# Attention, a token MLP and a top-1 mixture of experts: the experts' h taken to its transposed form through DRAM and VectorE, with the second product two blocks behind the first

## The chip, the cores and the metric

The kernel runs on one core of a Trainium2 chip. The metric is device time in microseconds (us) from start to end of one execution; lower is better. One core has five engines with queues of their own: TensorE (PE; its weight loads are listed as PEld), VectorE (DVE), ScalarE (ACT), GpSimd (POOL) and SyncE (SP), which here only issues DMAs. DMAs are issued from SP, ACT and POOL and move between DRAM and the on-chip memory. Matrix products land in PSUM, eight banks of 128 x 512 floats called `ps`.

## The reference

Three stages in a row on 4608 tokens of width 512.

```python
attn_out = _attn_ref(q, k, v, phi)                    # stage A
x = attn_out.transpose(0, 2, 1, 3).reshape(4608, 512)
h = x @ w_in                                          # stage B: 512 -> 2048 -> 512
x = (h / (1 + exp(-1.702 * h))) @ w_out
logits = x @ w_gate                                   # stage C: 8 experts, one for each token
e_idx = argmax(logits, axis=1)
gate_w = softmax(logits)[arange(N), e_idx]
eom = sigmoid(x @ w_output_gate)
for e in range(8):
    mask = e_idx == e
    h = maximum(x[mask] @ w1[e], 0)                   # 512 -> 1024
    out[mask] = gate_w[mask] * eom[mask, e] * (h @ w2[e])    # 1024 -> 512
```

With the inputs of this case the experts get 576, 0, 1152, 576, 1696, 576, 0 and 32 tokens; in blocks of 128 that is 5, 0, 9, 5, 14, 5, 0 and 1, 39 blocks in all.

## The kernel before

Every float32 operand of a product is split into a high and a low part (fp32r), and each product is made as high x high + high x low + low x high: three matmuls where one would do.

Stage B runs over nine tiles of 512 tokens. Beside it GpSimd splits the weights of one expert in each tile (`split_chunk`), and SP stores the parts to a DRAM scratch, `wsplit` (`store_chunk`). The tokens' results are scattered to DRAM as records of 524 floats (x, the router's numbers, the token's index), sorted by expert.

Stage C, the expert stage, runs over the 39 blocks. The busiest expert comes first (14 blocks), then the others by number: blocks 0-13, 14-18, 19-27, 28-32, 33-37 and 38. For a block i:

- GpSimd loads the records (`load_block`: four DMAs for `crec`, one for `cmeta`), VectorE transposes them in 32 x 32 blocks (`dve_x_t`), ACT and VectorE write the high and the low part `cx` (`act_x_hi`, `dve_x_lo`).
- TensorE makes h in two halves of 512 columns, 12 matmuls each (`block_h`), tokens on the partitions, in banks 0 and 1. ACT applies the relu to the first half, VectorE to the second, into `ch`.
- TensorE transposes `ch`: eight 128 x 128 transposes into banks 3 and 4 (`h_transpose`). From there ACT copies the high part and VectorE subtracts the low part, into `chT` (`act_h_hi`, `dve_h_lo`).
- TensorE makes y with 24 matmuls (`block_y`), ACT scales it by the gate (`act_y`), GpSimd scatters it to the output (`scatter_out`).

TensorE's order within block i is written out by hand: h(i), y(i-1), transposes of h(i). Every other engine has its own order, in `act_block`, `dve_block` and `pool_block`. Blocks 0 to 2 stand ahead of the loop, mixed with the end of stage B: the last tile's logits, the routing on VectorE (`route1`, `route2`), the counts, and then on VectorE some forty small instructions that make the tables of blocks, experts and rows (semaphore `b_tbl`). Records from block 3 on can only be loaded when those tables are there. Eight paddings of 128 records are stored too (`pad`), half by SP, half by ACT.

`W` has two slots of one expert's split weights each. SP loads an expert as four DMAs of 2 MB, one after the other, each waited for (`load_expert`); from the third expert on it first waits until y of the last block of the expert two before is done (`c_y`).

The functions that the diff touches follow as they were.

Of the kernel before, what the change touches and what calls it, by code (L numbers as in the profile page):

```python
# [31 lines left out]
P = 128  # L32
# [9 lines left out]
DM = H * D  # L42
# [15 lines left out]
CH = 512  # L58
EW = K1 * F2
# [31 lines left out]
def build(nc, q, k, v, phi, w_in, w_out, w_gate, w_ogate, w1, w2, cst, out):  # L91
    xT_dram = nc.dram_tensor("xT_scratch", (DM, N), F32, kind="Internal").ap()
    rec_dram = nc.dram_tensor("record_scratch", (NREC, REC), F32, kind="Internal").ap()
    wsplit = nc.dram_tensor("expert_scratch", (NE, P, 4 * EW), F32, kind="Internal").ap()
# [11 lines left out]
    with ExitStack() as ctx:  # L106
# [9 lines left out]
        sb("to_512", [P, 96])  # L116
# [14 lines left out]
        sb("to_512_again", [P, 72])  # L131
# [57 lines left out]
        with ExitStack() as a:  # L189


            sbt(a, "over_xraw", [P, K1 * T])
            ch = sbt(a, "ch", [P, F2])
            chT = sbt(a, "chT", [P, 2, C2, P], F32R)
            cy = sbt(a, "cy", [P, 2, DM])


            crec = sbt(a, "crec", [P, 4, 4, P])
            cxT = sbt(a, "cxT", [P, DM])
            cx = sbt(a, "cx", [P, 2, K1, P], F32R)  # L200
            cmeta = sbt(a, "cmeta", [P, 4, META])
            cex = sbt(a, "cex", [P, 4, NE])
            csum = sbt(a, "csum", [P, 4, 4])
# [68 lines left out]
        b_end = sem("record_ends")  # L272
        b_tbl = sem("tables")
# [7 lines left out]
        c_rec = [sem(f"records_loaded{r}") for r in range(4)]  # L281
# [4 lines left out]
        c_hact = sem("relu_by_act")  # L286
        c_hdve = sem("relu_by_dve")
# [16 lines left out]
        def ring(i, r):  # L304

            return i // 4 + 1
# [6 lines left out]
        LAST_BANK = (3, 4, 5, 6)  # L313
        EARLY = 3

# [22 lines left out]
        def blocks(eng, body, drain=None):  # L338


            n = (FULL - 3) // 4
            with eng.Fori(0, n) as m:
                for j in range(4):
                    body(4 * m + 3 + j, (3 + j) % 4)
            for i in range(3 + 4 * n, FULL):
                body(i, i % 4)
            used = eng.value_load(tbl[0:1, 5, 1:2], min_val=FULL, max_val=NBLK)
            for i in range(FULL, NBLK + 1):
                if i < NBLK:
                    with eng.If(used > i):  # L350
                        body(i, i % 4)
                if drain:
                    with eng.If(used == i):
                        drain(i, i % 4)
# [20 lines left out]
        def _(sp):  # L375
# [75 lines left out]
            def store_chunk(e, i):  # L451
                wait(sp, e_lo, 16 * e + i + 1)
                col = i * CH if i < 8 else 2 * EW + (i - 8) * CH
                for src, o in ((whi[:, i % 2, :].bitcast(F32), col), (raw[:, i % 2, :], col + EW)):
                    sp.dma_start(wsplit[bass.ds(e, 1), :, o:o + CH].rearrange("e p f -> p (e f)"), src
# [28 lines left out]
            def load_expert(e, j, chunks=range(4)):  # L484

                for n in chunks:
                    c_wn, c_n = (c_w1, 2 * j + n % 2 + 1) if n < 2 else (c_w2, 2 * j + n % 2 + 1)
                    col = n * EW
                    sp.dma_start(W[:, (j % 2) * SLOT + col:(j % 2) * SLOT + col + EW].bitcast(F32),
                                 wsplit[bass.ds(e, 1), :, col:col + EW].rearrange("e p n -> p (e n)")).then_inc(c_wn, 16)  # L490
# [1020 lines left out]
```

## Time and profile before

| | us |
|---|---|
| median of 3 runs | 1479.16 (1473.66 to 1483.98) |
| the profiled execution, its own time | 1479.53 |
| its span, first to last instruction | 1477.9 |
| TensorE busy in the span | 1407.9 (95%) |
| VectorE / ACT / GpSimd busy | 578.0 / 420.2 / 520.3 |
| stage C, from h of block 0 (993.2) to the end | 484.7 |

Starts are in us from the span's start. "L691" is line 691 of the kernel before: L691 is h, L720 is y, L731 the transposes of h, L612 and L646 are the two products of stage B. Matmuls are pipelined, so that the busy time of one (0.39 us) is longer than the distance of two starts; what a group of matmuls costs is read here from start to start. "Landing" is the time from a DMA's issue to its arrival.

### The profile page before, as it was taken

The numbers are of one execution on the slowest core, as the hardware profiler recorded it, in microseconds if no ns is written. First come the engines' busy times: TensorE is split into PE (matmuls) and PEld (weight loads), VectorE is DVE, ScalarE is ACT, GpSimd is POOL, SyncE is SP. The second block draws the span as 40 slices with busy tenths as digits, with TensorE's granted clock in tenths as the row PEclk, the third lists the DMA queues.
The fourth block names the chain that finished last, engine by engine and source line by source line (L and its number), as shares of the span: only waits on it lengthen the run. The fifth ranks groups of instructions, "written<-read, shape, count | busy, mean of one in ns | idle before, by whom it ended". The sixth has DMA issues, their size and how long they took to land.

```text
span 1477.9 us, 26796 instructions
## 1 busy us (share of the span) xinstructions
PE 1407.9 (95%) x8362; PEld 1145.9 (78%) x8363; DVE 578.0 (39%) x1254; ACT 420.2 (28%) x792; POOL 520.3 (35%) x617
## 2 busy tenths in 40 slices
PE   5777799999999999999999999998999999999997
PEld 4555578888888888888888888886888888888885
DVE  4777723334253342433334334236233233222331
ACT  3444422223222232222222322222222222222221
POOL 1121384435444344342533434013233333333332
PEclk9899999999999999999999999999999999999999
DMA  9999745555554545444453443326511265416371
GB/s 251 277 293 288 227 152 188 178 178 194 172 205 162 171 150 190 144 170 144 169 192 137 168 154 97 114 99 238 187 44 43 81 234 184 133 43 213 112 263 30
DMA packets 102359, 246.39 MB, mean 167 GB/s; under 512 B 16003, under 2 KB 16276, under 8 KB 99236
## 3 DMA queue, kind: packets, MB, share of 16 engines
q1 hardware_dynamic: 80404, 195.79, 40.3%
q0 software_dynamic: 13280, 32.09, 6.9%
q10 hardware_dynamic: 8624, 17.85, 3.5%
q8 instruction: 30, 0.49, 0.1%
q14 instruction: 21, 0.17, 0.0%
HBM read 146.00 MB, written 100.45 MB: 167 GB/s over the span
## 4 chain that ended last, share of the span: by engine, by line
PE 86%; DMA 7%; DVE 3%; SPq 2%; issue 1%; ACT 0%; POOL 0%; POOLq 0%; DVEq 0%
PE ps L612 27%; PE ps L646 26%; PE ps L691 14%; PE ps L720 14%; DMA qraw<-in_q 4%; DMA ph<-in_phi 2%; PE ps L731 2%; SPq L392 1%; PE ps L572 1%; PE ps L660 1%; PE ps L670 1%; DMA cmeta<-record_scratch 0%; PE ps L546 0%; DVE xs L1081 0%; PE ps L560 0%
## 5 line engine op out<-in xcount | busy, mean ns | idle before, releaser
L612 PE MATMUL ps<-xs,W 128*128 (+1 forms) x1728 | 422.7, 393 | 3.4 <-DVE xs L1081 3.4
L646 PE MATMUL ps<-W,gs 128*128 128x512 f32 x1728 | 415.1, 389 | 0.1
L612 PEld LDWEIGHTS ps<-xs,W 128*128 128x128 f32 x1728 | 321.6, 188 | 71.6 <-DVE xs L1081 4.0
L646 PEld LDWEIGHTS ps<-W,gs 128*128 128x128 f32 x1728 | 324.3, 188 | 67.8 <-DVE gs L1136 0.5
L1134 DVE TENSOR_TENSOR gate<-ps,gate 128x512 f32<-128x512 f32 x144 | 99.6, 691 | 401.4 <-ACT gate L887 400.9
L691 PE MATMUL ps<-W,cx 128*128 (+1 forms) x936 | 225.8, 397 | 4.7 <-DVE cx L1224 4.7
L720 PE MATMUL ps<-W,chT 128*128 (+1 forms) x936 | 218.9, 389 | 1.9 <-issue 1.9
L887 ACT ACTIVATE gate<-ps 128x512 f32<-128x512 f32 x144 | 86.1, 598 | 425.0 <-PE ps L612 412.8
L691 PEld LDWEIGHTS ps<-W,cx 128*128 128x128 f32 x936 | 174.8, 190 | 40.5 <-issue 5.2
L720 PEld LDWEIGHTS ps<-W,chT 128*128 128x128 f32 x936 | 175.6, 188 | 38.5 <-issue 2.1
L1412 POOL CAST whi<-raw 128x512 fp32r<-128x512 f32 x128 | 84.8, 663 | 305.0 <-DMA raw<-in_moe_w 304.9
L1414 POOL TENSOR_TENSOR raw<-raw,whi 128x512 f32<-128x512 f32 x128 | 172.3, 1346 | 21.5 <-POOL whi L1412 19.1
L1136 DVE TENSOR_TENSOR gs<-gate,gs 128x512 fp32r<-128x512 f32 x144 | 116.3, 808 | 100.2 <-ACT gs L891 99.5
L1426 POOL DMA_DIRECT2D crec<-record_scratch x164 | 92.4, 563 | 151.3 <-DMA out<-cy,cmeta 128.5
L891 ACT CAST gs<-gate 128x512 fp32r<-128x512 f32 x144 | 89.4, 621 | 112.8 <-DVE gate L1134 110.6
L1243 DVE TENSOR_TENSOR chT<-ps,chT 128x512 fp32r<-128x512 f32 x78 | 50.2, 686 | 180.4 <-ACT chT L934 180.3
L1467 POOL DMA_INDIRECT out<-cy,cmeta x39 | 40.6, 1041 | 166.5 <-ACT cy L941 157.3
L1420 POOL DMA_INDIRECT record_scratch<-rec,posi x36 | 36.5, 1013 | 152.4 <-DVE posi L1189 144.0
L941 ACT ACTIVATE cy<-ps,csum 128x512 f32<-128x512 f32 x39 | 26.8, 688 | 188.3 <-PE ps L720 186.8
L1238 DVE TENSOR_SCALAR ch<-ps 128x512 f32<-128x512 f32 x39 | 27.0, 691 | 105.8 <-PE ps L691 105.8
L1397 POOL CAST W<-raw 128x512 fp32r<-128x512 f32 x16 | 10.3, 644 | 132.0 <-DMA raw<-in_moe_w_in 132.0
L913 ACT CAST cx<-cxT 128x512 fp32r<-128x512 f32 x40 | 24.8, 621 | 80.3 <-PE ps L691 76.9
(159 smaller groups left out, 972.2 us busy)
## 6 DMA issues: line engine op xcount, KB each, us to landing
W<-expert_scratch SPq DMA_DIRECT2D x24, 2048.0 KB, 8.0
raw<-in_moe_w SPq DMA_DIRECT2D x128, 256.0 KB, 2.8
expert_scratch<-whi SPq DMA_DIRECT2D x128, 256.0 KB, 2.5
expert_scratch<-raw SPq DMA_DIRECT2D x128, 256.0 KB, 2.7
crec<-record_scratch POOLq DMA_DIRECT2D x164, 64.0 KB
kvm<-in_k SPq DMA_DIRECT2D x32, 288.0 KB, 5.6
kvm<-in_v SPq DMA_DIRECT2D x32, 288.0 KB, 9.8
qraw<-in_q SPq DMA_DIRECT2D x16, 576.0 KB, 14.0
```

The lines of the kernel that those rows point to most:

```text
L612: mm = pe.matmul(ps[:, f % 2, :], W[:, col:col + P], xs[:, bass.ds(x0 + (x_lo * K1 + c) * T, T)], start=(c == 0 and w_lo + x_lo == 0), sto ...
L646: mm = pe.matmul(ps[:, 2 + s, :], gs[:, f % 2, g_lo, s * P:(s + 1) * P], W[:, col:col + DM], start=(f == 0 and g_lo + w_lo == 0), stop=(f ...
L691: mm = pe.matmul(ps[:, j, :], cx[:, x_lo, c, :], W[:, bass.ds(col, 512)], start=(c == 0 and x_lo + w_lo == 0), stop=(c == K1 - 1 and x_lo ...
L720: mm = pe.matmul(ps[:, 5 + r % 2, :], chT[:, h_lo, c, :], W[:, bass.ds(col, DM)], start=(c == 0 and h_lo + w_lo == 0), stop=(c == C2 - 1 a ...
L887: act.activation(gate[:, f % 2, :], ps[:, f % 2, :], ACT.Sigmoid, scale=QTOK).then_inc(b_sig, 1)
L891: act.copy(gs[:, f % 2, 0, :], gate[:, f % 2, :]).then_inc(b_ghi, 1)
L1134: dve.tensor_tensor(gate[:, f % 2, :], ps[:, f % 2, :], gate[:, f % 2, :], ALU.mult).then_inc(b_g, 1)
L1136: dve.tensor_tensor(gs[:, f % 2, 1, :], gate[:, f % 2, :], gs[:, f % 2, 0, :].bitcast(F32), ALU.subtract).then_inc(b_glo, 1)
L1243: dve.tensor_tensor(chT[:, 1, 4 * j:4 * j + 4, :].rearrange("p c n -> p (c n)"), ps[:, 3 + j, :], chT[:, 0, 4 * j:4 * j + 4, :].rearrange( ...
L1412: pool.tensor_copy(whi[:, u, :], raw[:, u, :]).then_inc(e_hi, 1)
L1414: pool.tensor_tensor(raw[:, u, :], raw[:, u, :], whi[:, u, :].bitcast(F32), ALU.subtract).then_inc(e_lo, 1)
L1426: pool.dma_start(crec[b * M:(b + 1) * M, r], rows[:, b * P:(b + 1) * P].rearrange("(h n) d -> n h d", n=M)).then_inc(c_rec[r], 16)
```

## The change

- h goes through DRAM. The relu writes `ch` in another order of columns, `act_h_store` stores it (512 KB, 1 KB runs) to one of three places in `h_dram`, ACT waits for that, and `act_h_load` loads it back into `cq` with four tokens' quarters to a partition. VectorE transposes it in 32 x 32 blocks (`dve_h_t`, two of 512 columns) into `cqT`, from which ACT and VectorE write the parts `chT`. TensorE's eight transposes are gone.
- The second product is two blocks behind: TensorE's block is h(i), y(i-2). `chT`, `cx` and h's banks are double (banks 0, 1 and 3, 4). Before the loop the order is h0, h1, h2, y0, y1, y2, h3, h4.
- The rings of `cmeta`, `cex` and `csum` have six places, that of `crec` three; loops over blocks are unrolled by six. Record loads no longer wait for the last scatter.
- Loads of records 3 and 4 wait for a part of the tables only (`b_rows`), and stand ahead of `scatter_out(0)`. SP stores six of the eight paddings, ACT two.
- `wsplit` is laid out in pieces of 128 x 512, so that stores are contiguous and an expert's load has runs of 2 KB. SP may load w1 of a later expert when h, not y, of the old one is done.

```diff
@@ build
-    wsplit = nc.dram_tensor("expert_scratch", (NE, P, 4 * EW), F32, kind="Internal").ap()
+    wsplit = nc.dram_tensor("expert_scratch", (NE, 4, EW // CH, P, CH), F32, kind="Internal").ap()
+    h_dram = nc.dram_tensor("h_scratch", (3, 4, P, F2 // 4), F32, kind="Internal").ap()
@@ sync
-            for e in range(0, NE, 2):
+            for e in range(NE - 2):
                 pad(sp, e)
...
                         done = sp.value_load(tbl[0:1, 4, j:j + 1], min_val=1, max_val=NBLK)
+                        sp.wait_ge(c_h, done * 2)
+                    load_expert(e, j, range(2))
+                    if j >= 2:
                         sp.wait_ge(c_y, done)
-                    load_expert(e, j)
+                    load_expert(e, j, range(2, 4))
@@ tensor
             def pe_block(i, r):
-                block_h(i)
-                block_y(i - 1, (r - 1) % 4)
-                h_transpose(i)
+                block_h(i, r % 2)
+                block_y(i - 2, (r - 2) % RING)
@@ scalar
+            def act_h_store(i, n):
+                for j in range(2):
+                    wait(act, c_relu[j], i + 1)
+                act.dma_start(h_dram[n].rearrange("b p f -> p b f"), ch[:].rearrange("p (b f) -> p b f", b=4)).then_inc(c_hst, 16)
+
+            def act_h_load(i, n, u):
+                wait(act, c_hst, 16 * (i + 1))
                 wait(act, c_htr, 2 * i)
-                act.activation(ch[:, 0:512], ps[:, 0, :], ACT.Relu).then_inc(c_hact, 1)
-
-            def act_h_hi(i):
+                act.dma_start(cq[:], h_dram[n].rearrange("b (n h) f -> (b n) (h f)", h=4)).then_inc(c_hld[u], 16)
...
             def act_block(i, r):
-                act_relu(i)
+                act_relu(i, r % 2)
                 if not isinstance(i, int) or i + 1 < NBLK:
-                    act_x_hi(i + 1)
-                    act_exp(i + 1, (r + 1) % 4)
-                act_y(i - 1, (r - 1) % 4)
-                act_h_hi(i)
+                    act_x_hi(i + 1, (r + 1) % 2)
+                act_h_store(i, r % 3)
+                if not isinstance(i, int) or i + 1 < NBLK:
+                    act_exp(i + 1, (r + 1) % RING)
+                act_h_hi(i - 1, (r - 1) % 2)
+                act_h_load(i, r % 3, r % 2)
+                act_y(i - 2, (r - 2) % RING)
@@ vector
             def dve_block(i, r):
-                dve_relu(i)
+                dve_relu(i, r % 2)
                 if not isinstance(i, int) or i + 1 < NBLK:
-                    dve_x_lo(i + 1)
-                    dve_scale(i + 1, (r + 1) % 4)
-                dve_h_lo(i)
+                    dve_x_lo(i + 1, (r + 1) % 2)
+                    dve_scale(i + 1, (r + 1) % RING)
+                dve_h_t(i - 1, (r - 1) % 2)
+                dve_h_lo(i - 1, (r - 1) % 2)
```

TensorE from the end of stage B to the loop, before (L691 h, L761 and L670 the last tile's transposes and logits, L677 and L678 the counts, L720 y, L731 the transposes of h):

```order
L691 MATMUL ps<-W,cx 128x512 x24
L761 MATMUL ps<-ident,rec 128x128 x16
L670 MATMUL ps<-xraw,wg 32x128 x16
L731 MATMUL ps<-ident,ch 128x128 x8
L691 MATMUL ps<-W,cx 128x512 x12
L677 MATMUL ps<-hotb,before 128x128
L678 MATMUL ps<-hotb,ones 128x128
L691 MATMUL ps<-W,cx 128x512 x12
L720 MATMUL ps<-W,chT 128x512 x24
L731 MATMUL ps<-ident,ch 128x128 x8
L691 MATMUL ps<-W,cx 128x512 x24
L720 MATMUL ps<-W,chT 128x512 x24
```

The same stretch now (L705 h, L764 and L684 the transposes and logits, L691 and L692 the counts, L734 y):

```order
L705 MATMUL ps<-W,cx 128x512 x24
L764 MATMUL ps<-ident,rec 128x128 x16
L684 MATMUL ps<-xraw,wg 32x128 x16
L705 MATMUL ps<-W,cx 128x512 x12
L691 MATMUL ps<-hotb,before 128x128
L692 MATMUL ps<-hotb,ones 128x128
L705 MATMUL ps<-W,cx 128x512 x36
L734 MATMUL ps<-W,chT 128x512 x72
L711 TENSOR_LOAD tbl
```

All of h0 to h2 now stands ahead of y0, then y0 to y2 follow in one row; h3 and h4 come behind the TENSOR_LOAD.

ACT in one block behind the loop, before (L927 relu, L913 high part of cx, L921 exp of the gate, L941 scaling of y, L934 high part of h):

```order
L927 ACTIVATE ch<-ps 128x512
L913 CAST cx<-cxT 128x4x4x32
L921 ACTIVATE cex,csum<-cmeta 128x8
L941 ACTIVATE cy<-ps,csum 128x512
L934 CAST chT<-ps 128x512 x2
```

The same block now (L935 relu, L919 cx, L941 store of h, L927 exp, L954 high part of the h of the block before, L947 load of h, L962 scaling of y):

```order
L935 ACTIVATE ch<-ps 128x4x4x32
L919 CAST cx<-cxT 128x4x128
L941 DMA h_scratch<-ch 128x4x256
L927 ACTIVATE cex,csum<-cmeta 128x8
L954 CAST chT<-cqT 128x2x8x32 x2
L947 DMA cq<-h_scratch 128x1024
L962 ACTIVATE cy<-ps,csum 128x512
```

Two DMAs were added to ACT's queue, and ACT waits ahead of the second for the landing of the first.

VectorE now, between the tables and the loop (L1281 the last step of a gate's scale, L1267 transpose of records, L1286 relu, L1272 low part of cx, L1295 transposes of h, L1301 low part of h):

```order
L1267 STREAM_TRANSPOSE cxT<-crec 128x512
L1286 TENSOR_SCALAR ch<-ps 128x4x4x32
L1272 TENSOR_TENSOR cx<-cxT,cx 128x4x128
L1279 TENSOR_SCALAR csum<-csum 128x1
L1280 RECIPROCAL csum<-csum 128x1
L1281 TENSOR_TENSOR csum<-csum,cmeta 128x1
L1295 STREAM_TRANSPOSE cqT<-cq 128x512 x2
L1301 TENSOR_TENSOR chT<-cqT,chT 128x2x8x32 x2
```

The low part of the next block's x (L1272) stands behind the relu (L1286), which waits for the whole h of the block before it.

## Rows read from the trace of the kernel before

**Rows 1.** Page, chain that ended last, by line, shares of the span.

```profile
PE ps L612 27%; PE ps L646 26%; PE ps L691 14%; PE ps L720 14%; DMA qraw<-in_q 4%; DMA ph<-in_phi 2%; PE ps L731 2%; SPq L392 1%; PE ps L572 1%; PE ps L660 1%; PE ps L670 1%; DMA cmeta<-record_scratch 0%; PE ps L546 0%; DVE xs L1081 0%; PE ps L560 0%
```

**Rows 2.** Windows: stretch, length, busy of PE PEld DVE ACT POOL, clock, DMA share, GB/s.

```profile
1055.00:1443.00 388.00, 388.00 (x1846) 323.73 (x1845) 120.16 (x263) 100.61 (x228) 128.60 (x200) 1.00 0.39 132
```

**Rows 3.** Timeline of TensorE, one block of the loop: start, length, line, count.

```profile
1095.53 5.73 PE L691 MATMUL ps<-W,cx 128*128 x24
1101.10 5.61 PE L720 MATMUL ps<-W,chT 128*128 x24
1106.54 1.03 PE L731 MATMUL ps<-ident,ch 128*128 128x128 f32 x8
1107.33 2.98 PE L691 MATMUL ps<-W,cx 128*128 x12
```

**Rows 4.** Timeline of TensorE ahead of the loop; idle time before in brackets.

```profile
993.21 5.61 PE L691 MATMUL ps<-W,cx 128*128 128x512 f32 x24
998.65 1.91 PE L761 MATMUL ps<-ident,rec 128*128 128x128 f32 x16
...
1002.56 1.09 PE L731 MATMUL ps<-ident,ch 128*128 128x128 f32 x8
...
1033.78 8.51 PE L691 MATMUL ps<-W,cx 128*128 x24 [4.73 <-DVE cx L1224]
1042.13 5.61 PE L720 MATMUL ps<-W,chT 128*128 x24
```

**Rows 5.** Instructions of L731: count, shortest/median/longest in ns, first and last start.

```profile
L731 PE MATMUL ps<-ident,ch x312: 270/272/329, 1002.6 to 1461.0; 128*128 128x128 f32 x156
```

**Rows 6.** Timeline, the end: the last product and ACT's scaling of it.

```profile
1463.13 5.75 PE L720 MATMUL ps<-W,chT 128*128 x24 [1.86 <-issue]
1468.92 0.69 ACT L941 ACTIVATE cy<-ps,csum 128x512 f32<-128x512 f32 x1 [6.83 <-PE ps L720]
```

**Rows 7.** DMA issues: count, KB each, median us to landing.

```profile
W<-expert_scratch SPq DMA_DIRECT2D x24, 2048.0 KB, 8.0
...
qraw<-in_q SPq DMA_DIRECT2D x16, 576.0 KB, 14.0
xT_scratch<-xo ACTq DMA_DIRECT2D x16, 576.0 KB, 9.2
```

**Rows 8.** The transfers that write or read xT_scratch.

```profile
DMA to landing us min/median/max: 2.9/8.9/11.2
```

**Rows 9.** VectorE in 1055:1443, groups: busy us, mean ns, idle before.

```profile
L1243 DVE TENSOR_TENSOR chT<-ps,chT 128x512 fp32r<-128x512 f32 x66 | 42.5, 686 | 165.7 <-ACT chT L934 165.7
L1219 DVE STREAM_TRANSPOSE cxT<-crec 128x512 f32<-128x512 f32 x33 | 23.2, 704 | 11.8 <-DMA cmeta<-record_scratch 11.4 <-issue 0.3
```

**Rows 10.** ACT in 1055:1443, groups.

```profile
L934 ACT CAST chT<-ps 128x512 fp32r<-128x512 f32 x66 | 35.2, 590 | 0.0
L941 ACT ACTIVATE cy<-ps,csum 128x512 f32<-128x512 f32 x33 | 22.7, 688 | 158.5 <-PE ps L720 158.5
```

**Rows 11.** Windows ahead of the loop, columns as in rows 2.

```profile
1012.00:1018.00 6.00, 5.06 (x25) 3.68 (x24) 5.69 (x20) 1.84 (x5) 1.55 (x2) 1.00 1.01 373
...
1030.00:1036.00 6.00, 2.22 (x5) 1.82 (x6) 3.61 (x8) 1.78 (x5) 2.06 (x4) 0.74 0.90 300
1036.00:1042.00 6.00, 6.00 (x20) 4.71 (x19) 0.00 (x0) 0.60 (x1) 1.55 (x3) 0.69 0.66 222
```

**Rows 12.** Timeline of VectorE: steps of the tables, and the relu of block 3.

```profile
1014.00 0.51 DVE L1323 TENSOR_TENSOR xraw<-small,xraw 1x344 f32<-1x344 f32 x1
...
1015.21 0.50 DVE L1327 TENSOR_REDUCE xraw<-xraw 1x43 f32<-1x344 f32 x1
...
1017.28 0.17 DVE L1333 TENSOR_SCALAR xraw<-xraw 1x43 f32<-1x43 f32 x1
...
1020.36 0.07 DVE L1354 MEMSET small<- 128x8 f32 x1
...
1042.33 0.69 DVE L1238 TENSOR_SCALAR ch<-ps 128x512 f32<-128x512 f32 x1 [6.41 <-PE ps L691]
```

More of the change, by code:

```diff
@@ L58 @@
 CH = 512
+RING = 6
 EW = K1 * F2
@@ L280, in build @@
         c_w2 = sem("expert_w2_loaded")
-        c_rec = [sem(f"records_loaded{r}") for r in range(4)]
+        c_rec = [sem(f"records_loaded{r}") for r in range(RING)]
         c_xtr = sem("records_transposed")
@@ L285, in build @@
         c_h = sem("expert_h")
-        c_hact = sem("relu_by_act")
-        c_hdve = sem("relu_by_dve")
+        c_relu = [sem(f"relu_half{j}") for j in range(2)]
+        c_hst = sem("expert_h_stored")
+        c_hld = [sem(f"expert_h_loaded{u}") for u in range(2)]
         c_htr = sem("expert_h_transposed")
@@ L304, in ring @@
         def ring(i, r):
-            return i // 4 + 1
+            return i // RING + 1
         STEPS = C1
@@ L311, in build @@
         FULL = N // P
[L313 removed]
+        LAST_BANK = (2, 3, 4, 5)
         EARLY = 3
+        APART = EARLY + 2
         def pad(eng, e):
@@ L338, in blocks @@
         def blocks(eng, body, drain=None):
-            n = (FULL - 3) // 4
+            n = (FULL - APART) // RING
             with eng.Fori(0, n) as m:
[L343 to L346, printed above, removed]
+                for j in range(RING):
+                    body(RING * m + APART + j, (APART + j) % RING)
+            for i in range(APART + RING * n, FULL):
+                body(i, i % RING)
             used = eng.value_load(tbl[0:1, 5, 1:2], min_val=FULL, max_val=NBLK)
@@ L685, in block_h_half @@
                     wait(pe, c_xlo, i + 1)
-                    wait(pe, c_hact, i)
-                    wait(pe, c_hdve, i)
+                    for n in range(2):
+                        wait(pe, c_relu[n], i - 1)
                 for c in range(K1):
@@ L964, in act_tile @@
                             eom(t - 1)
-                        if last and f == 14:
-                            act_x_hi(0)
+                        if last and f >= 14:
+                            act_x_hi(f - 14, f - 14)
                     if not last and 11 <= f < 11 + K1:
@@ L994, in _ @@
+            for j in range(2):
+                act_relu(1, 1, j)
+            act_h_store(1, 1)
+            act_h_hi(0, 0)
+            act_h_load(1, 1, 1)
+            act.wait_ge(b_end, 1)
+            pad(act, NE - 2)
+            for j in range(2):
+                act_relu(2, 0, j)
+            act_h_store(2, 2)
+            pad(act, NE - 1)
+            act_h_hi(1, 1)
+            act_h_load(2, 2, 0)
             act_y(0, 0)
-            act_h_hi(1)
-            act_relu(2)
+            act_h_hi(2, 0)
@@ L1264, in dve_tile @@
                         dve_x_t(0, 0)
-                    if last and f == 14:
-                        dve_x_lo(0)
-                        dve_x_t(1, 1)
+                    if last and f >= 14:
+                        dve_x_lo(f - 14, f - 14)
+                        dve_x_t(f - 13, f - 13)
             tiles(dve, dve_tile)
             y_out(NT - 1)
-            dve_relu(0)
+            dve_relu(0, 0)
             for s in range(2, SUB):
```

224 lines of the change are left out of this document (131 added, 93 removed).

## The prediction

> **What bounds the kernel now.** I read the chain that ended last first, then the stretch of the loop in the windows, then TensorE's timeline. The chain is TensorE's almost throughout, and the h, y and transpose lines of the expert stage hold 14%, 14% and 2% of the span [rows 1]. In the loop TensorE is busy for 388 of 388 us at the full granted clock, while VectorE, ACT and GpSimd are each busy for a third at most and the DMA engines for 0.39 [rows 2]. So the stage goes by TensorE's own stream. One block is 5.57 us for h, 5.44 for y and 0.79 for the eight transposes, start to start, 11.80 in all (11.79 over many blocks) [rows 3]. An instruction taken out of this stream is a gain of its start-to-start time, one added to another engine costs nothing until it makes TensorE wait.
>
> **What is removed.** The transposes are 312 in 39 blocks [rows 5]; they take 0.79 us in a block. They cost a little more: h takes 5.57 us when it follows them, and 5.44 when it follows a matmul of 512 columns (h0, 993.21 to 998.65) [rows 3, 4]. So I take 5.44 for every product and 10.89 for a block, 0.90 less. If the 0.12 does not belong to the transposes it comes back, 36 x 0.12 = 4.3 us.
>
> **The sum.** Up to the logits nothing on TensorE changes. They ended when the first transposes began, at 1002.56 [rows 4]. There h1 starts now. Its halves take 5.44, the counts between them 0.1, and small steps about 0.2 more, then h2 another 5.44, so y0 starts at about 1013.8. From there 39 y and 36 h are left: 75 x 5.445 = 408.4, which ends at 1422.2 if nothing waits. Behind the start of the last y the trace has 5.44 + 9.33 us: 1463.13 to 1477.9 = 14.77 [rows 6]. So 9.3 follow the last product, and the idle 1.86 ahead of it goes too, if the last h is ready in time (below). Without any wait the span is 1431.5.
>
> **Waits in the loop: none in the sum.** Count from the start of h(i). It ends at 5.4; VectorE's relu begins 0.2 later and takes 0.69 [rows 12]. ACT issues the store at about 6.4. For the landing no row has this transfer. Nearest is the store of 576 KB from ACT in stage A, 9.2 us by the median, and 2.9 for the quickest transfer of that tensor, 11.2 for the slowest [rows 7, 8]; those slow ones ran beside SP's transfers. In a loop whose DMA engines are at 0.39 I take 3.5 for each way, and 6 to 9 beside a weight load. So h is back on chip at about 14 (quiet). VectorE takes it up in the next block, behind relu, cx and scale, at 10.9 + 7.9 = 18.8: two transposes of 0.70, then two parts of 0.59 on ACT and two of 0.69 on VectorE, partly side by side [rows 9, 10], done at 21.5. y(i) starts at 5.44 x 5 = 27.2. That leaves 6 us of slack, and the load may land 5 us later than VectorE is free without touching it. VectorE gets 1.4 us a block more work, 3.7 to 5.1 of 10.9; ACT two DMA issues. The new strides of cx and ch are priced by no row; were each of these four writes twice as long, VectorE would be at 6.5 of 10.9, still hidden. The same slack covers the end: h(38) lands while y(36) and y(37) run (10.9 us). In stage B the stores to `wsplit` change their layout only, behind a TensorE that is busy throughout: nothing.
>
> At one place the pages speak against the change. ACT's store shares the DMA engines with weight loads of 2 MB, 8.0 us each [rows 7], now in 2 KB runs. The Trainium skill (DMA: Bandwidth & Descriptors, section Queues, rings and completion order) says that a DMA engine drains a whole packet, typically 9-17 descriptors, from one queue before it turns to the next. By that page a store of 32 runs for each engine would wait behind two to four packets of 18 to 34 KB, 2 to 8 us over the quiet time. No row shows the packets of such a pair; the third rival below has the time for it, from rows.
>
> **Waits ahead of the loop: 14.7 us.** Here the profile is tight, and this is the part I know least.
> - y1 needs h1's way through DRAM. h1 ends at 1008.3, the store goes at 1009.1. Paddings and record scatters run then, and in 1012:1018 the DMA engines were at 1.01 of their time even before [rows 11]. At 2.9 each way with 0.6 for an issue, and 3.4 for transposes, parts and the two reductions in between, h1 is ready at 1019.5; y0 ends at 1019.2: 0.3 us. At 9.2 each way it is 12.9. I take 5.
> - y2 needs h2, whose low part stands behind the rest of the tables: 1.7 and 3.1 us of small steps (1014.00 to 1015.71, 1017.28 to 1020.4) [rows 12], about 0.5 for a scale, 1.4 for the transposes, 1.3 for the parts, 8 us after h1's. y1 covers 5.44: 2.6, and up to 5 if the store and load of h2 are slow too. I take 3.5.
> - h4 and h5 now follow h3 and h4 directly, and each needs cx, whose low part VectorE makes behind the relu of the h before: 0.2 + 0.69 + 0.69 + 0.14 = 1.7 us, twice: 3.4.
> - The clock. After an idle time of 4.73 us the next 24 matmuls took 8.35 us instead of 5.57, with a granted clock of 0.74 and 0.69; after 1.86 us they took 5.75, no loss [rows 4, 6, 11]. The wait for y1 is nearer to the first: 2.8 us, between 0 and 5.6 if it happens twice.
>
> What goes in return: the idle 4.73 us and the slow 2.8 ahead of h3 [rows 4]. They don't stand in the new sum, since records 3 and 4 are asked for before the tables are complete, and y1 and y2 stand ahead of h3 and cover their loads.
>
> Span: 1431.5 + 5 + 3.5 + 3.4 + 2.8 = 1446.2. The profiled execution took 1.6 us more than its span, and its 1479.5 is at the median of the runs (1479.16). So 1447.8; I say **1447**, 2.1% less than before.
>
> **Rivals.**
> - *Forecast, 0.70:* TensorE's stream of 10.9 us a block and 7 to 25 us of waits ahead of the loop: 1438 to 1457.
> - *Cleaner start, 0.06:* DRAM's way costs h1 nothing, and h4 and h5 find cx ready: 1431.5 + 2.6 + 1.6, about 1436. VectorE's order speaks against it.
> - *Weight loads hold up h, 0.18:* ACT waits for its store's landing in its queue. From that landing to the next store it has a load to issue, a scaling, a relu and a cx, about 2.5 us, so its cycle is landing + 2.5. At 9.2 that is 11.7, 0.8 over TensorE's 10.9, and with three blocks to a weight load the slack of 6 holds. At 11.2 it is 2.8 over, 8.4 in three blocks, 2.4 beyond the slack, five times: +12, 1459, and with a slow start up to 1468. For it: the transfers from ACT in stage A. Against it: SP has one weight load in flight at a time here, and in stage A had five transfers. The page's packets end here too: 2.9 + 8 = 11.
> - *Slower than before, 0.04:* the same mechanism at the 14.0 us of SP's q loads [rows 7]: cycle 16.5, 16.8 over in three blocks, 10.8 beyond the slack, five times, +54: 1501. It decides from a landing of about 12.7 us on: 32 us to lose in five loads are 6.4 each and the slack of 6, 4.1 a block.
> - *No gain, 0.02:* some other queue (GpSimd's loads and scatters) sets a period of 11.8 us: 1479.
>
> **Numbers.** A difference of 1% is about what this measurement can tell from none, so faster is below 1464, slower above 1494. Faster: forecast, cleaner start and five sixths of the weight rival, 0.91. Same: the rest of that and half the last, 0.05. Slower: 0.04. The range leaves out the lowest tenth and what lies above the middle of the weight rival: 1436 to 1462. The forecast's own is 1438 to 1457.
>
> **What would show it.** Right: in the loop TensorE's starts of h are 10.9 us apart, busy 100% of the time; L731's rows are gone; 2 to 6 us idle ahead of y1, some ahead of y2, 1.7 ahead of h4 and of h5. Idle time of TensorE that returns beside weight loads, with ACT waiting for `h_scratch`, shows the third case. The store's landing is the number to look at first: above 9 us in the loop my slack is wrong. If h still takes 5.57, the 0.12 was not the transposes'.

## The result, and the profile after

The changed kernel takes 1462.01 us (median of 20 runs, 1450.76 to 1472.83) against 1473.71 us for the kernel before (20 runs, 1464.68 to 1483.98). The ratio of the means is 0.9917, 95% interval 0.9889 to 0.9944, where one slow run of the changed kernel (1472.83) is left out. So it is faster, by 0.8%; the prediction had 1447 us, 2.1% less than the 1479.16 that three runs had given for the kernel before. The runs of the two kernels spread over 19 and 22 us, and that is stage A's: over the profiles of this text the first product of stage B starts between 157.7 and 176.3 us, and from there to h0 it is 817.3 to 819.2. The profiles are therefore compared by the expert stage alone, from the first matmul of h0 to the end: 484.7 us before, 471.3 after, where the prediction's own sum gives 1446.2 - 993.2 = 453.0.

The page of the changed kernel, the chain by line (L705 is h, L734 is y) and DMA issues with their median landing:

```profile
PE ps L626 27%; PE ps L660 27%; PE ps L705 11%; PE ps L734 9%; DMA h_scratch<-ch 6%; DMA ph<-in_phi 3%; DMA qraw<-in_q 2%; DMA cmeta<-record_scratch 1%; SPq L403 1%; PE ps L674 1%; PE ps L586 1%; DMA W<-expert_scratch 1%; PE ps L684 1%; SPq L426 0%; PE ps L574 0%
...
W<-expert_scratch SPq DMA_DIRECT2D x24, 2048.0 KB, 11.9
...
h_scratch<-ch ACTq DMA_DIRECT2D x39, 512.0 KB, 4.1
cq<-h_scratch ACTq DMA_DIRECT2D x39, 512.0 KB, 3.5
```

The transposes are gone from the chain [rows 1], and 6% of the span is now h's store in that chain, which did not exist before. Weight loads land in 11.9 us instead of 8.0 [rows 7]. The stretch of rows 2 now reads:

```profile
1055.00:1443.00 388.00, 376.18 (x1637) 308.50 (x1637) 186.23 (x345) 126.16 (x241) 127.93 (x199) 0.99 0.72 236
```

TensorE is no longer busy throughout, VectorE went from 120 to 186 us, the DMA engines from 0.39 to 0.72. A quiet block, and the stretch ahead of the loop, in TensorE's timeline:

```profile
1009.30 5.60 PE L734 MATMUL ps<-W,chT 128*128 128x512 f32 x24
1019.20 7.14 PE L734 MATMUL ps<-W,chT 128*128 128x512 f32 x24 [4.30 <-DVE chT L1301]
1027.47 5.70 PE L734 MATMUL ps<-W,chT 128*128 128x512 f32 x24 [1.13 <-issue]
1033.01 5.60 PE L705 MATMUL ps<-W,cx 128*128 x24
1040.53 5.75 PE L705 MATMUL ps<-W,cx 128*128 x24 [1.91 <-DMA W<-expert_scratch]
1048.33 7.34 PE L705 MATMUL ps<-W,cx 128*128 x24 [2.05 <-DVE cx L1272]
1055.51 5.60 PE L734 MATMUL ps<-W,chT 128*128 x24
...
1111.78 5.60 PE L734 MATMUL ps<-W,chT 128*128 x24
1117.22 5.60 PE L705 MATMUL ps<-W,cx 128*128 x24
1122.66 5.60 PE L734 MATMUL ps<-W,chT 128*128 x24
...
1185.40 7.33 PE L705 MATMUL ps<-W,cx 128*128 x24 [2.07 <-DVE cx L1272]
1192.57 5.60 PE L734 MATMUL ps<-W,chT 128*128 x24
...
1244.72 7.04 PE L705 MATMUL ps<-W,cx 128*128 x24 [2.85 <-DVE cx L1272]
```

Without a wait a block takes 10.88 us (1111.78 to 1122.66) where it took 11.80 [rows 3]. But the loop has seven idle times, 11.75 us together, and two of them are followed by a slow stretch: after 2.07 us the next 24 matmuls take 7.17 us from start to start, not 5.44. By stretches, predicted (from the terms of the sum) against measured:

| stretch | predicted | measured |
|---|---|---|
| h0 to y0 | 20.6 | 20.64 |
| y0 to y3, six products and the waits ahead of the loop | 47.4 | 46.21 |
| y3 to the end of y38, 69 products of 5.445 | 375.7 | 392.64 |
| end of y38 to the end | 9.3 | 11.85 |
| stage | 453.0 | 471.3 |

The missing 18 us are in the loop, 16.9, and behind it, 2.5. What stands ahead of the loop came out 1.2 us better than predicted.

**Where the loop's waits come from.** Each one is beside weight loads or a few us behind them, and TensorE waits for cx, the split and transposed tokens of the next block, not for h. One of them, in the timeline of all engines (L947 is ACT's load of h, L962 the scaling of y, L1540 GpSimd's scatter, L1498 and L1500 its record loads, L1267 VectorE's transpose of records, L1272 the low part of cx):

```profile
1226.72 0.33 ACTq L947 DMA_DIRECT2D cq<-h_scratch  x1
...
1227.28 0.69 ACT L962 ACTIVATE cy<-ps,csum 128x512 f32<-128x512 f32 x1 [5.26 <-DMA h_scratch<-ch]
...
1228.90 1.04 POOL L1540 DMA_INDIRECT out<-cy,cmeta  x1 [8.29 <-ACT cy L962]
...
1232.39 2.47 POOL L1498 DMA_DIRECT2D crec<-record_scratch  x4 [2.45 <-issue]
...
1237.31 2.36 POOL L1498 DMA_DIRECT2D crec<-record_scratch  x4 [0.43 <-issue]
...
1241.63 0.71 DVE L1267 STREAM_TRANSPOSE cxT<-crec 128x512 f32<-128x512 f32 x1 [7.85 <-DMA cmeta<-record_scratch]
...
1243.50 1.08 DVE L1272 TENSOR_TENSOR cx<-cxT,cx 128x512 fp32r<-128x512 f32 x1 [0.59 <-ACT cx L919]
```

ACT stands 5.26 us idle until h's store has landed (that store had been issued at 1215.73, 11.0 us before), then issues the load and only then scales y. GpSimd's scatter has waited 8.29 us for that, and the record loads stand behind the scatter in GpSimd's queue. VectorE waits 7.85 us for records and makes cx 1.2 us ahead of TensorE's late h. The record loads themselves took 4.6 to 6.7 us there, where 2.2 is the median of a quiet stretch (1085 to 1140), and their issue came 2.45 us behind the scatter for no reason that the profile shows.

Four of the seven waits (1185.40, 1244.72, 1346.32, 1404.47; 8.4 of the 11.75 us) end this way, with VectorE 6.6 to 7.9 us idle for records. The other three (1084.45, 1172.17, 1391.48; 3.3 us) end on a shorter one. The first of them:

```profile
1078.99 0.71 DVE L1267 STREAM_TRANSPOSE cxT<-crec 128x512 f32<-128x512 f32 x1 [4.25 <-DMA cmeta<-record_scratch]
...
1081.06 0.69 ACT L962 ACTIVATE cy<-ps,csum 128x512 f32<-128x512 f32 x1 [7.04 <-DMA h_scratch<-ch]
1081.64 0.59 ACT L935 ACTIVATE ch<-ps 128x512 f32<-128x512 f32 x1
1082.12 1.09 ACT L919 CAST cx<-cxT 128x512 fp32r<-128x512 f32 x1
...
1083.24 1.07 DVE L1272 TENSOR_TENSOR cx<-cxT,cx 128x512 fp32r<-128x512 f32 x1 [2.06 <-ACT cx L919]
```

Here the records are transposed in time. ACT's own half of cx (L919) is late, because it stands behind the wait for the store, the scaling and the relu, and TensorE starts h at 1084.45.

In all, the waits of the stretch 1055 to 1443 (who waited for whom, us, times, longest) are:

```profile
ACT cy L962 <- DMA h_scratch<-ch: 64.9, 12, 7.5
DVE cxT L1267 <- DMA cmeta<-record_scratch: 61.7, 18, 7.8
```

Before, VectorE waited 11.4 us for records [rows 9]. This is the theory to be tested, **the queue theory**: ACT holds y's scaling behind the wait for h's store, and the delay goes by GpSimd's queue to cx. **The bandwidth theory** is its rival: record loads land late because the DMA engines are full, whatever the order. Both need the weight loads; they differ in whether late landings alone are enough.

### The profile page after: what moved, and what is told of

Same layout as the page of the kernel before. It is cut to its first block, busy times and chain, and to the rows that moved or that the text cites. A ratio compares the mean times of both kernels' runs of the same rounds, so it can differ in the third digit from the quotient of the medians.

```text
span 1460.0 us, 26488 instructions
## 1 busy us (share of the span) xinstructions
PE 1379.4 (94%) x8050; PEld 1114.3 (76%) x8051; DVE 644.4 (44%) x1331; ACT 446.2 (31%) x794; POOL 517.5 (35%) x617
## 3 DMA queue, kind: packets, MB, share of 16 engines
q10 hardware_dynamic: 34544, 58.21, 11.5%
## 4 chain that ended last, share of the span: by engine, by line
PE 77%; DMA 12%; DVE 3%; issue 3%; SPq 2%; ACT 1%; ACTq 0%; POOLq 0%; POOL 0%; DVEq 0%
PE ps L626 27%; PE ps L660 27%; PE ps L705 11%; PE ps L734 9%; DMA h_scratch<-ch 6%; DMA ph<-in_phi 3%; DMA qraw<-in_q 2%; DMA cmeta<-record_scratch 1%; SPq L403 1%; PE ps L674 1%; PE ps L586 1%; DMA W<-expert_scratch 1%; PE ps L684 1%; SPq L426 0%; PE ps L574 0%
## 5 line engine op out<-in xcount | busy, mean ns | idle before, releaser
L705 PE MATMUL ps<-W,cx 128*128 (+1 forms) x936 | 224.7, 397 | 15.8 <-DVE cx L1272 10.6
L734 PE MATMUL ps<-W,chT 128*128 (+1 forms) x936 | 219.8, 391 | 5.4 <-DVE chT L1301 4.3
L705 PEld LDWEIGHTS ps<-W,cx 128*128 128x128 f32 x936 | 178.1, 191 | 57.5 <-issue 20.5
L734 PEld LDWEIGHTS ps<-W,chT 128*128 128x128 f32 x936 | 176.6, 189 | 43.0 <-issue 6.2
L1540 POOL DMA_INDIRECT out<-cy,cmeta x39 | 40.7, 1045 | 248.0 <-ACT cy L962 247.1
L1498 POOL DMA_DIRECT2D crec<-record_scratch x164 | 91.7, 560 | 55.5 <-issue 49.7
L954 ACT CAST chT<-cqT 128x512 fp32r<-128x512 f32 x78 | 47.0, 621 | 86.4 <-DVE cqT L1295 86.4
L1286 DVE TENSOR_SCALAR ch<-ps 128x512 f32<-128x512 f32 x37 | 25.3, 685 | 103.2 <-PE ps L705 99.8
L1295 DVE STREAM_TRANSPOSE cqT<-cq 128x512 f32<-128x512 f32 x78 | 50.9, 691 | 29.8 <-DMA cq<-h_scratch 24.0
L962 ACT ACTIVATE cy<-ps,csum 128x512 f32<-128x512 f32 x39 | 26.9, 689 | 101.7 <-DMA h_scratch<-ch 64.9
L1267 DVE STREAM_TRANSPOSE cxT<-crec 128x512 f32<-128x512 f32 x41 | 29.1, 709 | 65.2 <-DMA cmeta<-record_scratch 64.9
## 6 DMA issues: line engine op xcount, KB each, us to landing
W<-expert_scratch SPq DMA_DIRECT2D x24, 2048.0 KB, 11.9
```

Of the source, the lines that this page charges most:

```text
L705: mm = pe.matmul(ps[:, 3 * u + j, :], cx[:, u, x_lo, c, :], W[:, bass.ds(col, 512)], start=(c == 0 and x_lo + w_lo == 0), stop=(c == K1 - ...
L734: mm = pe.matmul(ps[:, 5 + r % 2, :], chT[:, r % 2, h_lo, c, :], W[:, bass.ds(col, DM)], start=(c == 0 and h_lo + w_lo == 0), stop=(c == C ...
L1295: dve.transpose(cqT[:, j * 512:(j + 1) * 512], cq[:, j * 512:(j + 1) * 512]).then_inc(c_htr, 1)
L1498: pool.dma_start(crec[b * M:(b + 1) * M, r % 3], rows[:, b * P:(b + 1) * P].rearrange("(h n) d -> n h d", n=M)).then_inc(c_rec[r], 16)
```

## The experiments

All figures are of one profile each, in us: the stage (484.7 before the change), y0 to y3, and y3 to the end of y38 (375.7 without a wait); the ratio is to the kernel before. yfirst_b is the kernel of yfirst, profiled a second time.

| kernel | stage | y0 to y3 | y3 to end of y38 | ratio [95%] |
|---|---|---|---|---|
| changed | 471.3 | 46.2 | 392.6 | 0.992 [0.989, 0.994] |
| noweights | 455.9 | 48.0 | 375.4 | 0.982 [0.976, 0.987] |
| yfirst | 457.7 | 48.7 | 376.8 | 0.984 [0.979, 0.990] |
| yfirst_b | 457.7 | 48.3 | 377.3 | 0.979 [0.975, 0.983] |
| scatter3 | 464.0 | 52.3 | 378.9 | 0.989 [0.983, 0.994] |
| runs16k | 465.9 | 50.4 | 382.3 | 0.988 [0.982, 0.995] |
| cxfirst | 460.7 | 48.3 | 380.1 | 0.983 [0.977, 0.989] |
| latepads | 472.7 | 50.5 | 389.7 | 0.989 [0.982, 0.997] |
| cx16k | 475.8 | 51.8 | 392.1 | 0.987 [0.981, 0.994] |
| yfirst16k_b | 466.6 | 51.9 | 381.7 | 0.987 [0.983, 0.992] |
| lateweights_b | 450.4 | 40.6 | 377.4 | 0.976 [0.972, 0.980] |
| shorttail_b | 455.6 | 46.9 | 378.1 | one run only |

### Is it the weight loads? noweights

```diff
+                    if j:
+                        sp.dma_start(W[:, (j % 2) * SLOT + col:(j % 2) * SLOT + col + 16].bitcast(F32),
+                                     wsplit[bass.ds(e, 1), n, 0, :, 0:16].rearrange("e p f -> p (e f)")).then_inc(c_wn, 16)
+                    else:
...
```

> The changed kernel, but of the experts after the first only 16 columns of each quarter of their weights are loaded (so those experts' products are left out in substance; every other instruction stays). In the changed kernel's profile TensorE waits for cx five or six times behind the start of the loop, each time beside weight loads (h of later blocks at 1084, 1185, 1244, 1346, 1391, 1404 us), and y3 to y38 with h6 to h38 take 392.6 us instead of 69 x 5.445 = 375.7. Theory of both kinds (the weight loads are what stretches the loop): no TensorE wait in the loop, that stretch 376 us, 16 to 17 us less; h's store lands in under 4.5 us throughout. Rival: the waits come from the loop's own queues (GpSimd's loads and scatters, VectorE's longer cx), then they stay, at least in part, above 385 us.

Measured: y3 to the end of y38 375.4 us, no idle time of TensorE in it. h's transfers land in 2.8/3.1/6.8 us (shortest, median, longest), record loads in 3.3 at most. The loop's own queues are fast enough; all of the 16.9 us need the weight loads. That does not tell the two theories apart.

### Is it what ACT holds back? yfirst

```diff
                 act_h_hi(i - 1, (r - 1) % 2)
-                act_h_load(i, r % 3, r % 2)
                 act_y(i - 2, (r - 2) % RING)
+                act_h_load(i, r % 3, r % 2)
```

> The changed kernel with one edit: in ACT's block the scaling of y(i-2) stands ahead of the load of h(i), which waits for the landing of h(i)'s store. Queue theory: beside weight loads the store lands late (up to 12.5 us), ACT holds the scaling of y behind that wait, GpSimd's scatter waits for the scaling and the next record load stands behind the scatter in GpSimd's queue, so VectorE gets the records late and TensorE waits for cx. Then this edit takes most of the loop's 16.9 us of waits away: stretch y3 to y38 at 376 to 380 us, 0.8 to 1.1% faster than the changed kernel. Bandwidth theory: the record loads land late because the DMA engines are full, wherever the scaling stands: stretch stays at 388 to 394 us and the time within 0.3% of the changed kernel's.

Measured: 376.8 us, and 377.3 in a second profile. Two instructions exchanged in one queue took 15 to 16 of the 16.9 us away. The weight loads and h's traffic are as before, h's transfers as late (10.6 us at most, 12.5 in the second profile), and so are the record loads (7.5 and 7.8 at most). VectorE's wait for records in the same stretch:

```profile
DVE cxT L1267 <- DMA cmeta<-record_scratch: 17.3, 13, 4.1
```

61.7 us became 17.3. So record loads are not slow enough in themselves to hold TensorE; the bandwidth theory falls. ACT still waits for the store, but what stands behind the wait is now the load of h, the next relu and its half of cx, which come 0.6 us earlier than behind the scaling. The shorter way to cx is still there: the one wait for cx in the second profile (0.44 us at 1086.61) ends on it, with the records transposed 5 us before.

### Which link? scatter3

```diff
             def pool_block(i, r):
                 if not isinstance(i, int) or i + 2 < NBLK:
                     load_records(i + 2, (r + 2) % RING)
-                scatter_out(i - 2, (r - 2) % RING)
+                scatter_out(i - 3, (r - 3) % RING)
```

> The changed kernel with one edit: GpSimd's scatter of y stands one block later (y(i-3) in block i), so that a record load is no longer queued behind the scatter of a y whose scaling ACT may still hold back. ACT's order is the changed kernel's, so ACT still waits for h's store ahead of the scaling (64.9 us in all in the changed kernel). Queue theory: the link that hurts is scatter before record load in GpSimd's queue. Then VectorE's waits for records (61.7 us) fall below 25, TensorE's waits for cx in the loop go, y3 to y38 take 376 to 380 us, as with the scaling moved. If instead late relus on ACT are what holds cx up, the loop's waits stay near 17 us. Bandwidth theory (record loads slow in themselves): stays too.

Scatter 2 is moved behind record load 6 in the same way, and the last scatters follow at the end. Measured: y3 to the end of y38 378.9 us. ACT's waits ahead of the scaling are unchanged, but VectorE's wait for records is down (26.0, where I had written below 25):

```profile
ACT cy L962 <- DMA h_scratch<-ch: 65.7, 17, 7.7
DVE cxT L1267 <- DMA cmeta<-record_scratch: 26.0, 11, 5.0
```

The delay on ACT is there in full and hurts little once the scatter ahead of a record load is that of an older y, whose scaling is done. That is the link, and it holds although the edit adds a wait of its own: the place in the ring of `cmeta` that a record load writes is now the one whose scatter was issued just before, so GpSimd waits for that scatter to land (1055 to 1430; the changed kernel has no such row):

```profile
POOL crec L1498 <- DMA out<-cy,cmeta: 157.3, 30, 9.4
```

The two waits that are left in the loop (1.05 and 1.06 us, at 1229.91 and 1384.00) end on the shorter way, ACT's own cx. The stage gained only 7.3 us, because h5 waited 5.4 us for cx ahead of the loop. That was not GpSimd's order, for its records were transposed in time. h3's store, issued at 1038.13 beside a weight load issued at 1037.96, came back 10 us later, and the relus of h4 waited for it to free `ch`, ahead of cx (ACT in 1030 to 1430):

```profile
ACT ch L935 <- DMA h_scratch<-ch: 14.5, 2, 10.1
```

### Long or short runs? runs16k, before2k, yfirst16k_b, cx16k

Each has, against the kernel that it starts from (the changed kernel, the kernel before, yfirst and cxfirst), the other layout of the expert weights and nothing else: `wsplit` as (expert, 128, 16384) with loads of 16 KB runs in the changed kernel's variants, as (expert, 4, 8, 128, 512) with 2 KB runs in the kernel before.

> The kernel before with only the new layout of the expert weights (2 KB runs). TensorE was busy throughout the loop, so the time stays within 0.3% of before's. The landing of a 2 MB weight load without h's traffic tells what of 11.9 us the short runs cost: 8.0 to 8.5 if the h traffic is the cause, 10 or more if the runs are.

Measured: 0.995 [0.992, 0.999], a little more than the 0.3% that I allowed; the stage 482.1 us against 484.7, because h3 waited 3.48 us instead of 4.73 ahead of the loop; in the loop TensorE has no idle time in either. A weight load landed in 9.4 us by the median, where the kernel before had 8.0 [rows 7] and the changed kernel 11.9. So the short runs alone are 1.4 of the 3.9 us that it got longer, and neither 8.0 to 8.5 nor 10 or more was right. The next run completes the four cases: with long runs h's traffic adds 0.7 us (8.7), with short runs 2.5 (11.9). The two do not simply add up.

> The changed kernel with the expert weights in the old layout of DRAM (16 KB runs in a load, 64 KB pitch in a store); nothing else. If the 2 KB runs make the weight loads long (8.0 us before, 11.9 in the changed kernel) and hold up nothing, the loads get back towards 9 and the loop's waits shrink. If, as the change supposes, short runs let the small transfers of h and of the records in between, then h's store and the record loads land later here beside weight loads (over 12 us) and the loop's waits grow beyond 16.9 us, time 1 to 3% above the changed kernel's. I expect the second, more weakly: 1 to 2%.

Measured: the opposite of what I expected, 465.9 us, less waiting in the loop (6.6 instead of 16.9 us). Weight loads landed in 8.7 us, so the time in which they can disturb is shorter by a quarter; that this is the reason is not shown. The gain of 5.4 us is from one profile of each, and the ratios of the whole time, 0.988 and 0.992, do not tell the two kernels apart.

> yfirst with the expert weights in the old layout (16 KB runs). So far the two layouts gave opposite answers: the stage was 5 us shorter with long runs in the changed kernel's order, 15 us longer in cxfirst's, where y waited for h in five places. In the order of yfirst nothing is queued behind the store's landing but the load and the next relu. If long runs delay single transfers of h (store or load at 9 to 12 us), y3 and two or three later y wait, stage 460 to 468; if the two answers were the order's doing and chance, the stage is 456 to 459.

Measured: 466.6, against 457.7 twice with short runs; on one chip the medians are 1456.66 and 1445.17 us. With the queue in order, long runs cost 9 us: 4.7 in the loop (381.7 against 377.0), 3.4 ahead of it (51.9 against 48.5) and 1 in the tail. y now waits for h in the loop. Four of TensorE's waits behind y3, in the timeline:

```profile
1171.92 5.75 PE L735 MATMUL ps<-W,chT 128*128 x24 [0.31 <-DVE chT L1302]
1227.04 5.72 PE L735 MATMUL ps<-W,chT 128*128 x24 [0.41 <-DVE chT L1302]
...
1326.75 5.73 PE L735 MATMUL ps<-W,chT 128*128 x24 [0.42 <-DVE chT L1302]
1383.00 5.75 PE L735 MATMUL ps<-W,chT 128*128 x24 [1.55 <-DVE chT L1302]
```

So short runs are better with the scaling moved; in the changed kernel the one profile of each says the opposite. What short runs protect is not shown. The longest landing of h was 10.4 us with long runs and 10.6 and 12.5 with short ones; only VectorE's longest single wait for h's load was longer, 6.8 us against 5.1 and 4.9.

> cxfirst with the expert weights in the old layout (16 KB runs). With the changed kernel the old layout was no worse (weight loads 8.7 us instead of 11.9, the stage 465.9 instead of 471.3 us, ratio 0.988 against 0.992), against what I expected. If short runs cost nothing and bring nothing once the queues are in order: within 2 us of cxfirst in the stage and 0.3% in time. If they protect h's transfers: h's store and load wait longer beside weight loads and y waits for h here (over 3 us in the loop).

Measured: 475.8 us, 15 more than cxfirst, of which 12 in the loop: y waits for h in four places behind y3 (1.5 to 2.9 us) and y38 0.8 us, released by nothing the profile shows. This agrees with yfirst16k_b, but latepads below, with short runs and the same loop order as cxfirst, has 389.7 us in the loop too, so this pair alone would not have shown it.

### Ahead of the loop: cxfirst, latepads, lateweights_b

cxfirst puts the parts of cx of block i+1 ahead of the relu of block i, on both engines, on top of yfirst:

```diff
             def dve_block(i, r):
-                dve_relu(i, r % 2)
                 if not isinstance(i, int) or i + 1 < NBLK:
                     dve_x_lo(i + 1, (r + 1) % 2)
+                dve_relu(i, r % 2)
```

> The kernel with the scaling ahead of the load of h (as in the run yfirst) and, on ACT and VectorE, the parts of cx for block i+1 ahead of the relu of block i, in the loop and for blocks 4 and 5 ahead of it. If h4 and h5 wait (1.9 and 2.05 us, each followed by a slow stretch, 7.33 us for 24 matmuls instead of 5.60) only because the low part of cx stands behind the relu that waits for the whole h before it, then both waits and both slow stretches go: 7 us less of the expert stage than yfirst's 457.7, about 450, ratio to the kernel before 0.979 to 0.981. Rival: the records of block 4 and 5 are what is late (VectorE waited 3.3 us for them), then only part of it goes, stage at 453 to 456.

Measured: both waits and their slow stretches are gone, and the stage is 460.7, no better than yfirst. The timeline tells why:

```profile
1034.65 16.69 PE L705 MATMUL ps<-W,cx 128*128 x72
1058.98 8.30 PE L734 MATMUL ps<-W,chT 128*128 x24 [7.63 <-DVE chT L1301]
```

h3, h4 and h5 run without a break, and y3 waits 7.63 us for h3's way through DRAM, with a slow stretch behind it. h3's store is issued at 1041.07, just behind a weight load at 1040.91, and ACT issues the load of h3 only at 1051.48. The wait has only moved: neither of the two cases I had written down.

latepads adds to cxfirst `sp.wait_ge(c_hld[1], 16)` ahead of SP's paddings.

> cxfirst, and SP stores its six paddings only when h of block 1 is back from DRAM. y1 waited 4.3 to 4.7 us in three profiles, for h1's store and load (4.2 and 5.6 us) beside paddings and record scatters. If those DMAs are the cause, h1 takes 2 x 3.3 us, y1 waits 0 to 2 us and the slow stretch behind it goes; but records 3 need the paddings, so h3 may be late instead: net 0 to 4 us less than cxfirst. If the wait is ACT's and VectorE's order (relu, tables), y1 still waits 3 us or more.

Measured: y1's wait fell from 4.5 to 1.8 us, so SP's paddings, the only DMAs that were moved, were more than half of it. In exchange y2 waited 2.6, h3 3.6 and y3 5.6 us: nothing gained, y0 to y3 50.5 us. The loop lost 14 us here as well (with ACT's cx behind the wait for the store, 49.7 us of waiting); cxfirst's order in the loop is not a robust one.

lateweights_b keeps yfirst's loop, puts cx first for blocks 4 and 5 only, and holds the second expert's weights back:

```diff
+            sp.wait_ge(c_h, 12)
             for j in range(1, NE):
```

> The version meant to beat both: the scaling ahead of the load of h (yfirst), cx ahead of the relu for blocks 4 and 5 only, and SP starts the load of the second expert's weights when h5 is done instead of when the tables are. In cxfirst the waits of h4 and h5 (1.9 and 2.05 us with their slow stretches) were gone and y3 waited 7.6 us in their place, for h3's way through DRAM, which ran beside the first weight loads of the stage (that of the second expert, needed only at block 14). If those loads are the cause, y3 waits under 2 us here and the stage falls from 457.7 to about 449, ratio 0.978 to 0.981. If h3's way is long for ACT's or VectorE's own order, y3 waits 4 us or more and the stage stays at 455 or above.

Measured: 450.4 us, 1437.68 us by the median, 0.976 [0.972, 0.980]; it beats both kernels. Ahead of the loop only y1 waits:

```profile
1009.78 7.98 PE L735 MATMUL ps<-W,chT 128*128 128x512 f32 x24 [4.67 <-DVE chT L1302]
1018.04 5.71 PE L735 MATMUL ps<-W,chT 128*128 128x512 f32 x24 [0.29 <-issue]
1023.59 16.71 PE L706 MATMUL ps<-W,cx 128*128 x72
1040.13 5.66 PE L735 MATMUL ps<-W,chT 128*128 x24
```

y3 follows h5 without idle time, so its 7.6 us in cxfirst were the weight loads': ahead of y3 the two kernels differ in nothing else, and ACT issues the load of h3 2.8 us behind the store, not 10.4. In cxfirst those loads were started as soon as the tables were there, at 1028.9, for h14, which starts at 1154.2, 125 us later. Here they start at 1041.1 and h14 at 1133.4, still 92 us later.

> The kernel of yfirst once more, for its time beside lateweights on one chip and a second profile: 0.984 of the kernel before, stage 457 to 459 us, no wait of TensorE between y3 and y37 over 0.5 us.

Measured: stage 457.7 and no wait over 0.44 us between y3 and y37, as expected; the ratio 0.979 [0.975, 0.983], where I had written 0.984. On the same chip lateweights_b is 7.5 us faster (1437.68 against 1445.17, six runs each that spread over 18 and 13 us), as its stage is 7.3 us shorter.

### The tail: shorttail_b

> yfirst without the conditional bodies of blocks 40 to 42, which these inputs never enter (39 blocks); all that is computed here stays. All profiles of the changed shape have 11.1 to 12.4 us from the end of the last matmul to the end, the two of the old shape 9.0. If the rest is instruction fetch over the skipped bodies (5 instruction DMAs in the tail instead of 3), the tail falls to 10 us or less; if not it stays above 11.

```diff
-            for i in range(FULL, NBLK + 1):
+            for i in range(FULL, FULL + 5):
```

The conditional steps now end at 40 instead of 43. So it is the bodies of blocks 41 and 42, with three endings, that are gone; that of block 40 stays.

Measured: from the end of y38 to the end 10.1 us (11.3 to 12.6 in the other kernels of the changed shape, 9.2 before), with one packet of the instruction queues in it where yfirst_b has five and the kernel before three. Against yfirst and yfirst_b (11.6 and 11.5) these skipped steps cost about 1.5 us. This is one profile of one run, and the number of these bodies was the same in the kernel before, so why they cost more now stays open.

## Why the prediction was wrong

**Right, with its size.** TensorE's stream bounds the stage, and without a wait a block without transposes takes 10.88 us (10.89 predicted). The 0.12 us did belong to the transposes: h takes 5.44 us now. h0 to y0 was right to 0.1 us. Ahead of the loop, 13.5 us were lost (46.2 less six products) where 14.7 was the forecast: y1 4.30 + 1.55 of slow stretch (5 + 2.8), y2 1.1 (3.5), h4 and h5 1.9 and 2.05 with 1.74 of slow stretch (3.4), and 0.1 to 0.2 at each new start. The mechanism of h4 and h5 was as written: cxfirst removed both. That y1 waits for DMAs beside paddings was right too (latepads). That the sum came out within 1.2 us is partly luck: noweights, yfirst and yfirst_b have the same order ahead of the loop and took 48.0 to 48.7 us there, mostly because the idle 1.91 us ahead of h4 was followed by a slow stretch in them.

**Wrong: "Waits in the loop: none in the sum".** The landing itself was not misjudged: 3.5 us assumed when quiet, 3.3 measured (median of both ways, 1085 to 1140); 6 to 9 assumed beside a weight load, up to 12.5 measured, and h's own way had the slack of 6 us that I gave it: with yfirst, and stores that land as late, no y waits for h in the loop but the last, 1.1 us. So the sign that I had named, a store above 9 us, came true and pointed at the wrong slack. What failed is the step from the wait to its victims. I followed the h that waits, y(i) and its slack, and counted the scaling of y behind the wait as 0.69 us of ACT's cycle. I did not follow the scaling on: its scatter stands in GpSimd's queue ahead of the next record load, whose landing VectorE waits for in its own order, ahead of cx. I even noted that record loads no longer wait for the last scatter to land. They still wait for it to be issued. The shorter way I left out as well: the next block's cx stands on ACT behind the same wait, and nowhere in the sum is there a slack for cx. This term was put at nothing and measured 16.9 us.

**The third rival** (weight loads hold up h, 0.18, 1459 to 1468) had the place, the trigger and nearly the time: 1462 measured, on the upper end of the range. But its account was of ACT's cycle over three blocks against h's slack of 6, with y as what waits. The waits came at landings at which that sum still gave none, and for cx: ahead of the wait at 1244.72, ACT issued three loads of h 9.4, 11.0 and 4.1 us behind their stores, by that sum 3.6 us over and within the slack. It also took a weight load at 8.0 us, three blocks for the four of an expert; at 11.9 they are four and a half. The trace has a landing of 9.7 us over the quickest at most (12.5 less 2.8). The Trainium skill (DMA: Bandwidth & Descriptors, section Queues, rings and completion order) says that a DMA engine drains a whole packet from one queue before it turns to the next, and the prediction's estimate from it was 2 to 8 us. The direction agrees, and it deserved more weight; the longest landing lies above the estimate. No run here shows the packets themselves.

**Too small: the tail.** 9.3 was carried over, 11.85 measured, in every kernel of the new shape over 11 but shorttail_b; about 1.5 us are the skipped steps (above), the rest is open.

**Not in the sum: the strides of cx.** I called them priced by no row and hidden even at double. They were 1.07 us instead of 0.69 on VectorE and 1.09 instead of 0.62 on ACT, and hidden in quiet blocks; they make a late cx later by 0.4 and 0.5 us.

**The chances.** 0.91 for faster by over 1% rested on a range of loop waits that had one source. With the loop clean and the same order ahead of it (noweights) the stage is 455.9, so the forecast of 453.0 was a kernel in which all goes well. In the chances themselves the rest of the weight rival and half of the last are 0.04, not 0.05.

## What to carry to other kernels

- When a change puts a wait for a DMA into a compute engine's queue, list what is behind it in that queue, and for each entry who waits for it and what stands behind that one in its own queue. The slack to test is the smallest on any of these paths, not that of the data that waits. Put the wait last: the instructions that other queues live on go ahead of it.
- A bulk transfer that is started as early as possible takes bandwidth from transfers with a deadline. If it is needed 125 us later, hold it back past the tight place: `sp.wait_ge(c_h, 12)` together with the new order of two cx was 7 us.
- A wait that is removed uncovers the next one (h4, h5, then y3). Read the whole stretch before pricing a single wait.

## What the hardware showed that I had not expected

- The landing of a 512 KB store went from 2.8 to 12.5 us beside one 2 MB load of another queue, and a 2 MB load takes 8.0, 9.4, 8.7 or 11.9 us by the median: long runs alone, short runs alone, long and short runs beside h's traffic.
- Short idle times of TensorE can cost more than themselves. Idle times of 2.05, 2.07 and 2.85 us in the changed kernel were followed by 24 matmuls in 7.18, 7.17 and 6.88 us instead of 5.44; 1.1 to 1.83 us of idle cost 0.10 to 0.15. The length alone does not decide: 1.91 us cost 0.15 us in the changed kernel and 1.7 us in noweights and yfirst, and 2.94 us in cx16k (at 1233.79) cost 0.15, with a granted clock of 1.00 behind it. In the slow stretch behind 2.07 us the granted clock (the column ahead of the last two) was 0.76, so part of it ran at the lower of the two levels, 1.2 GHz, and the next stretch at 2.4 GHz again, as before the change [rows 11]:

```profile
1185.40:1192.60 7.20, 7.20 (x25) 5.79 (x26) 3.34 (x6) 3.48 (x5) 2.45 (x4) 0.76 0.89 312
1192.60:1200.00 7.40, 7.40 (x34) 6.15 (x33) 5.38 (x10) 2.13 (x5) 1.39 (x3) 1.00 0.75 256
```

- A write to on-chip memory with a step of four float elements took 1.09 us for 128 x 512 on ACT where runs of 32 elements took 0.62, and 1.07 against 0.69 on VectorE.
